# Three-stage kernel: the last expert tile's step takes over the preparation of the dense stage, and four smaller moves

## The chip, the cores and the metric

The kernel runs on one core of one Trainium2 chip, as one program. The metric is the device time of one execution in microseconds (us), and the median of three executions stands for the kernel. TensorE is called PE in the rows, VectorE DVE, ScalarE ACT, GpSimd POOL and SyncE SP. SP only issues transfers. "q" behind an engine's name means its sequencer, the part that reads instructions, tests conditions, loads registers and hands work to the engine.

## The reference

Three layers follow each other. Attention with a window of 16 positions and block summaries gives 1536 tokens of 512 values. A top-1 mixture of 8 experts takes each token through one expert. A dense layer with a squared ReLU ends it.

```python
def reference(**kwargs):
    ...
    attn_out = _attn_ref(**attn_kwargs)          # (2, 8, 768, 64), local window + block maxima and means
    x = attn_out.transpose(0, 2, 1, 3).reshape(B * S, H * D)     # 1536 x 512
    x = _moe_ref(x=x, **moe_kwargs)
    return _moe2_ref(x=x, **moe2_kwargs)

# experts: D 512, F 1024, E 8
logits = x @ w_gate + modality_bias[modality_id]
e_idx = argmax(logits); gate_w = softmax(logits)[e_idx]
out[mask] = gate_w[mask, None] * (relu(x[mask] @ w1[e]) @ w2[e])
# dense: 512 -> 2048 -> 512
h = relu(x @ w_in);  return (h * h) @ w_out
```

## The kernel before

**Stages.** Attention handles the 1536 tokens in 12 blocks of 128 (NB = 12, index i). While it ends, the tokens are routed: each block is scattered to a list of its expert in DRAM (`xs_d`). The expert stage then goes through tiles of 128 tokens, each of one expert; their number n_t is known only at run time (it was 13 in the profiled execution, from 13 times 8 matmuls of one line). The dense stage takes the tokens in 3 groups of 512.

**Precision.** Every fp32 operand is split in two parts, `high` (a copy by ACT) and `low` (the difference, by DVE or POOL), and each product is made of three matmuls. So weights that arrive in `raw` have to be split into `W` before PE can use them. W has two slots. A run is a row of tiles of one expert, and the runs take turns in the slots. The weights come in 8 parts of 512 KB, four of the first layer and four of the second (PARTS = 4). The dense stage's weights go the same way: `w_in` as if it was one more run, and `w_out` into the slot that the last expert leaves, first half (`out_high` and `out_low` of parts 0 to 3) before the dense stage, second half inside it where `swapped` is 0.

**A tile's step** on PE is `layer1(t)`, `x_transpose(t+1)`, `layer2(t-1)`, `h_transpose(t)`. The first three tiles (SPEC = 3) are written out, the others run in a loop of 9 rounds of two steps, each under a test `t < n_t`, on PE, ACT, DVE and SP alike. Rounds past n_t still are gone through, with both tests failing. A last `layer2(n_t - 1)` stands behind the loop. In such a step ACT makes ReLU, `x_high(t+1)`, the high part of h, stores the tile before (`ys_d`), and splits weights where the table says so (`split_next`, which loads a register from `table` and tests it). DVE makes `x_low(t+1)`, `y_copy(t-1)`, `h_low(t)`, and the low parts of weights (`low_next`, which loads and tests likewise).

**Tokens of the dense stage.** Group 0 is read back in four blocks, `z_part[0..3]`, of which the last two lie in `x_in` and are loaded once the last `x_transpose` has run. DVE multiplies each by its gate (`scale_parts`), PE transposes it (`part_transposes`), ACT and DVE split it into `z_hi` and `z_lo`. The first matmuls of the dense stage (`up(0, 0)`) wait for all four `z_lo`. `up(g, f)` is 12 matmuls, followed from f = 2 on by `down(g, f - 2)` of 12; ACT makes `r_sb` from each, DVE `sq`, ACT `s_hi`, DVE `s_lo`, for which `down` waits.

**Order.** Nothing is scheduled by a tool: every engine runs its own instruction list in the order in which it is written, and semaphores join them. Transfers of SP wait in SP's own order.

**The start of the expert stage.** SP loads the first expert's 8 parts of weights from attention's block 9 on. POOL scatters the blocks in five groups (`RGROUPS`); when groups 0 and 1 have landed it reads tiles 0 and 1 from `xs_d` (semaphores `s_x0`), and PE transposes tile 0. `tables()` on DVE makes all per-tile tables and raises `tab`; n_t is read from them. The first matmuls of tile 3 stand behind DVE's `x_low(3)`.

Of the kernel before, what the change touches and what calls it, by code (L numbers as in the profile page):

```python
# [5 lines left out]
F32 = mybir.dt.float32  # L6
# [8 lines left out]
P = 128  # L15
# [36 lines left out]
GT = 4  # L52
# [90 lines left out]
def build(nc, a):  # L143
# [257 lines left out]
    with block:  # L401

        @block.sync
        def _(sp):
# [46 lines left out]
            for i in range(VRING, NB):  # L451
# [35 lines left out]
            with sp.Fori(0, (TILES - SPEC) // 2) as m:  # L487
                for j in range(2):
                    t = m * 2 + (j + SPEC)
                    with sp.If(t < n_t):  # L490
                        moe_step(t, 1 - j)
# [25 lines left out]
        def _(act):  # L517
# [100 lines left out]

            def moe_step(t, s=None, before=None):
# [34 lines left out]
            n_run = n_r(act)  # L654
            with act.Fori(0, (TILES - SPEC) // 2) as m:
                for j in range(2):
                    t = m * 2 + (j + SPEC)
                    with act.If(t < n_t):
                        moe_step(t, j, m + (j + 2))


            swapped = act.snap((n_run + 1) & 1)

            def out_high(part):
                act.activation(Wv(swapped, 0, part * PW, PW), raw[:, part * PW:(part + 1) * PW], ACT.Copy
                               ).then_inc(sem["wo_h"], 1)

            def out_second(parts):
                act.wait_ge(sem["l2"], n_t)
                act.wait_ge(s_wo[1], 16)  # L670
                for part in parts:
                    out_high(part)
# [6 lines left out]
            for j in range(GT):  # L679
                act.wait_ge(sem["zt"], j + 1)  # L680
                act.activation(z_hi[:, :, j * P:(j + 1) * P], part_bank(j)[:, :].rearrange("p (k t) -> p k t", k=KD),
                               ACT.Copy).then_inc(sem["zh"], 1)
            act.wait_ge(sem["l1"], n_t * 2)
            act.wait_ge(s_wo[0], 16)
            for part in range(PARTS):
                out_high(part)
# [183 lines left out]
        def _(dve):  # L870
# [159 lines left out]
            for i in range(NB):  # L1030
# [19 lines left out]
                if i in (5, 6):  # L1050
                    sum_values(1, i - 3)
# [49 lines left out]

            T1 = TILES + 1
# [47 lines left out]
            def moe_step(t, s, lap):  # L1150
                x_low(t + 1)
                if isinstance(t, int) and t == 1:
                    dve.wait_ge(sem["scat_d"], RGROUPS[4][1] * 16)
                dve.wait_ge(s_ys[s], lap * 16 + 16)
                y_copy(t - 1, y_sb[s])
                if isinstance(t, int) and t == 1:
                    rows_of_tiles()
                if not isinstance(t, int):
                    with dve.If(t == last):
                        scale_parts(range(2))  # L1160
                h_low(t)
                if not isinstance(t, int):
# [3 lines left out]
            def scale_parts(js):  # L1166
                dve.wait_ge(sem["sorted"], 16)
                for j in js:
# [41 lines left out]
            dve.tensor_tensor(lsub[:, :, :], logit[:, :, :], wide(lmax[:, :], 2, E), ALU.subtract).then_inc(sem["lsub"], 1)  # L1210
# [17 lines left out]
            with dve.Fori(0, (TILES - SPEC) // 2) as m:  # L1228
                for j in range(2):
                    t = m * 2 + (j + SPEC)  # L1230
                    with dve.If(t < n_t):
                        moe_step(t, j, m + 1)
# [12 lines left out]
            swapped = dve.snap((n_run + 1) & 1)  # L1245

            def out_low(parts):
                for part in parts:
                    dve.wait_ge(sem["wo_h"], part + 1)
                    dve.tensor_tensor(Wv(swapped, 1, part * PW, PW), raw[:, part * PW:(part + 1) * PW],  # L1250
# [398 lines left out]
```

## Time and profile before

| what | us |
| --- | --- |
| median of 3 executions | 542.31 |
| lowest, highest | 540.24, 543.75 |
| the profiled execution, whole | 542.34 |
| its span, first to last instruction | 540.70 |
| PE busy in the span | 512.3 (95%) |
| DVE, ACT, POOL busy | 226.6, 186.5, 87.9 |
| mean granted clock of PE | 0.989 of full speed |

The profiled execution took what the median took, and 1.64 us of it lie outside its span. PE is busy in 95% of the span, but matmuls are pipelined and their ends are modelled, so the share alone doesn't tell how much could be won; the gaps between PE's instructions do.

### The profile page before, as it was taken

The page shows a single profiled execution, that of the slowest core. Times are in us where ns is not written, and L with a number is a line of the kernel's source. Part 1 is how long each engine was busy: PE and PEld are TensorE (multiplying, and loading weights), DVE is VectorE, ACT ScalarE, POOL GpSimd, SP SyncE. Part 2 cuts the span into 40 slices and gives each one's busy share as a digit, 9 for nine tenths or more (in the row PEclk, how much of TensorE's full clock was granted, in tenths as well). Part 3 has the DMA queues.
Part 4 walks back from the last instruction along what each step waited for, and adds up shares of the span by engine and source line. Part 5 has one row for each costly group of instructions (what it writes and reads, how often), then busy time and mean ns, then how long its engine had stood idle before and what let it go on. Part 6 is the DMA issues. An engine that isn't in the chain of part 4 may idle for free.

```text
span 540.7 us, 9465 instructions
## 1 busy us (share of the span) xinstructions
PE 512.3 (95%) x3118; PEld 412.9 (76%) x3119; DVE 226.6 (42%) x439; ACT 186.5 (34%) x353; POOL 87.9 (16%) x111
## 2 busy tenths in 40 slices
PE   8699989979999999997999999999999999999994
PEld 3477778867888888885788888888888888888883
DVE  3686676876312635312862322432332233222231
ACT  0856664315422545421641222332212133122220
POOL 4343335117530040400000000110000020000002
PEclk9989998999999999999999999999999999999998
DMA  8999882229491247531010000120000010000002
GB/s 295 299 269 292 245 287 112 80 52 359 65 334 50 78 178 290 175 133 58 31 68 0 1 1 1 69 86 0 0 0 0 0 58 19 0 0 0 0 0 78
DMA packets 18682, 54.92 MB, mean 102 GB/s; under 512 B 2768, under 2 KB 3040, under 8 KB 17888
## 3 DMA queue, kind: packets, MB, share of 16 engines
q1 hardware_dynamic: 10864, 27.47, 17.0%
q0 software_dynamic: 5200, 23.62, 12.1%
q10 hardware_dynamic: 2592, 3.49, 1.8%
q8 instruction: 15, 0.25, 0.2%
q14 instruction: 11, 0.09, 0.1%
HBM read 42.51 MB, written 12.07 MB: 101 GB/s over the span
## 4 chain that ended last, share of the span: by engine, by line
PE 85%; DVE 5%; issue 3%; DMA 2%; ACT 1%; DVEq 1%; POOL 0%; another core or an unknown queue 0%; POOLq 0%; SPq 0%; ACTq 0%
PE psum L1579 8%; PE psum L1580 8%; PE psum L1578 8%; PE psum L1595 8%; PE psum L1594 8%; PE psum L1596 8%; PE psum L1494 4%; PE psum L1493 4%; PE psum L1495 4%; PE psum L1473 4%; PE psum L1475 4%; PE psum L1474 4%; PE psum L1398 2%; PE psum L1503 2%; PE psum L1313 2%
## 5 line engine op out<-in xcount | busy, mean ns | idle before, releaser
L1268 DVE TENSOR_TENSOR sq<-r_sb 128x512 f32<-128x512 f32 x48 | 33.2, 692 | 137.0 <-ACT r_sb L694 137.0
L694 ACT ACTIVATE r_sb<-psum 128x512 f32<-128x512 f32 x48 | 28.7, 597 | 147.4 <-PE psum L1580 147.4
L1594 PE MATMUL psum<-W,s_hi 128*128 128x512 f32 x192 | 75.8, 395 | 0.0
L1579 PE MATMUL psum<-z_lo,W 128*128 128x512 f32 x192 | 75.8, 395 | 0.0
L1580 PE MATMUL psum<-z_hi,W 128*128 128x512 f32 x192 | 75.8, 395 | 0.0
L1578 PE MATMUL psum<-z_hi,W 128*128 128x512 f32 x192 | 75.7, 394 | 0.0
L1595 PE MATMUL psum<-W,s_hi 128*128 128x512 f32 x192 | 75.6, 394 | 0.0
L1596 PE MATMUL psum<-W,s_lo 128*128 128x512 f32 x192 | 75.3, 392 | 0.0
L860 POOL DMA_INDIRECT out<-o_sb,sorted_m x12 | 11.6, 968 | 297.8 <-ACT o_sb L706 294.8
L1270 DVE TENSOR_TENSOR s_lo<-sq,s_hi 128x512 fp32r<-128x512 f32 x48 | 33.3, 693 | 33.5 <-ACT s_hi L696 33.5
L1473 PE MATMUL psum<-W,x_hi 128*128 (+1 forms) x104 | 42.4, 407 | 1.8 <-issue 1.2
L696 ACT ACTIVATE s_hi<-sq 128x512 fp32r<-128x512 f32 x48 | 30.3, 632 | 38.9 <-DVE sq L1268 38.9
L1578 PEld LDWEIGHTS psum<-z_hi,W 128*128 128x128 f32 x192 | 36.0, 188 | 8.7
L1580 PEld LDWEIGHTS psum<-z_hi,W 128*128 128x128 f32 x192 | 36.0, 187 | 8.7
L1579 PEld LDWEIGHTS psum<-z_lo,W 128*128 128x128 f32 x192 | 36.0, 187 | 8.6
L1594 PEld LDWEIGHTS psum<-W,s_hi 128*128 128x128 f32 x192 | 36.1, 188 | 8.3
L1596 PEld LDWEIGHTS psum<-W,s_lo 128*128 128x128 f32 x192 | 36.1, 188 | 8.2
L1595 PEld LDWEIGHTS psum<-W,s_hi 128*128 128x128 f32 x192 | 36.1, 188 | 8.1
L1493 PE MATMUL psum<-W,h_hi 128*128 (+1 forms) x104 | 41.9, 403 | 0.0
L1475 PE MATMUL psum<-W,x_lo 128*128 (+1 forms) x104 | 41.2, 396 | 0.0
L1474 PE MATMUL psum<-W,x_hi 128*128 (+1 forms) x104 | 41.0, 394 | 0.0
L1494 PE MATMUL psum<-W,h_hi 128*128 (+1 forms) x104 | 40.9, 394 | 0.0
(204 smaller groups left out, 735.5 us busy)
## 6 DMA issues: line engine op xcount, KB each, us to landing
raw<-in_w POOLq DMA_DIRECT2D x4, 2048.0 KB
raw<-in_w_io POOLq DMA_DIRECT2D x4, 2048.0 KB, 8.1
v_in<-in_v SPq DMA_DIRECT2D x12, 390.0 KB, 9.3
raw<-in_w SPq DMA_DIRECT2D x8, 512.0 KB, 8.1
kT<-in_kT SPq DMA_DIRECT2D x8, 400.0 KB, 6.5
q_in<-in_q SPq DMA_DIRECT2D x12, 256.0 KB, 7.9
X<-in_vT SPq DMA_DIRECT2D x2, 1536.0 KB, 13.6
x_in<-xs_d SPq DMA_DIRECT2D x12, 256.0 KB
```

The lines of the kernel that those rows point to most:

```text
L1270: dve.tensor_tensor(s_lo[f % SBUFS][:, :], sq[:, :], s_hi[f % SBUFS][:, :].bitcast(F32), ALU.subtract).then_inc(sem["s_l"], 1)
L1473: pe.matmul(bank[h][:, :], x_hi[:, k, :], wh, start=(k == 0), stop=False)
L1474: pe.matmul(bank[h][:, :], x_hi[:, k, :], wl, start=False, stop=False)
L1475: ins = pe.matmul(bank[h][:, :], x_lo[:, k, :], wh, start=False, stop=(k == KD - 1))
L1493: pe.matmul(bank[4][:, :], h_hi[:, k, :], wh, start=(k == 0), stop=False)
L1494: pe.matmul(bank[4][:, :], h_hi[:, k, :], wl, start=False, stop=False)
L1578: pe.matmul(bank[f % 2][:, :], wh, z_hi[:, k, :], start=(k == 0), stop=False)
L1579: pe.matmul(bank[f % 2][:, :], wh, z_lo[:, k, :], start=False, stop=False)
L1580: ins = pe.matmul(bank[f % 2][:, :], wl, z_hi[:, k, :], start=False, stop=(k == KD - 1))
L1594: pe.matmul(bank[2 + j][:, :], s_hi[f % SBUFS][:, tok], wh, start=(f == 0), stop=False)
L1595: pe.matmul(bank[2 + j][:, :], s_hi[f % SBUFS][:, tok], wl, start=False, stop=False)
L1596: ins = pe.matmul(bank[2 + j][:, :], s_lo[f % SBUFS][:, tok], wh, start=False, stop=(f == KFF - 1))
```

## The change

It has six parts. (1) The last tile's step now holds, under a test `t == last`, what stood behind the loop: on ACT the high parts of group 0's tokens (`parts_high`) and of w_out's first half (`out_first`), on DVE the scaling of all four blocks ahead of `y_copy`, then their low parts, w_out's low parts and the copy of the last y. On PE all 16 transposes of the blocks stand ahead of the last `layer2`, where 8 stood ahead of it and 8 inside. (2) In the loop the second step's test is nested in the first's, so that a round past the end is left after one test. (3) SP issues parts 4 to 7 of the first expert's weights only once tile 1 (`s_x0[1]`) has landed. (4) PE transposes tile 3 inside `layer2(1)`, ahead of its seventh piece of eight, and reads n_t and n_run ahead of its eighth. (5) One reduction of v for the second batch (`sum_values(1, 3)`) moves on DVE from block 6 to block 5. (6) `lsub`, the input of ACT's exponentials of the gates, is computed ahead of the tables.

```diff
@@ SP
-                if i >= NB - RING:
+                if NB - RING <= i < NB - 1:
                     load_weights(e, (i - (NB - RING)) * 2)
-            load_weights(e, 2 * RING)
+            sp.wait_ge(s_x0[1], 16)
+            load_weights(e, PARTS)
+            load_weights(e, PARTS + 2)
@@ ACT
+            def out_first():
+                act.wait_ge(sem["l1"], n_t * 2)
+                act.wait_ge(s_wo[0], 16)
+                out_high(range(PARTS))
...
+            def parts_high():
+                for j in range(GT):
+                    act.wait_ge(sem["zt"], j + 1)
+                    act.activation(z_hi[:, :, j * P:(j + 1) * P], part_bank(j)[:, :].rearrange("p (k t) -> p k t", k=KD),
+                                   ACT.Copy).then_inc(sem["zh"], 1)
...
                 if not isinstance(t, int):
+                    with act.If(t == last):
+                        parts_high()
+                        out_first()
+                if not isinstance(t, int):
                     split_next(t - 1, 1)
                     split_next(t, 0)
...
             with act.Fori(0, (TILES - SPEC) // 2) as m:
-                for j in range(2):
-                    t = m * 2 + (j + SPEC)
-                    with act.If(t < n_t):
-                        moe_step(t, j, m + (j + 2))
+                t = m * 2 + SPEC
+                with act.If(t < n_t):
+                    moe_step(t, 0, m + 2)
+                    with act.If(t + 1 < n_t):
+                        moe_step(t + 1, 1, m + 3)
@@ DVE
-                if i in (5, 6):
-                    sum_values(1, i - 3)
+                if i == 5:
+                    sum_values(1, 2)
+                    sum_values(1, 3)
...
+            dve.tensor_tensor(lsub[:, :, :], logit[:, :, :], wide(lmax[:, :], 2, E), ALU.subtract).then_inc(sem["lsub"], 1)
             T1 = TILES + 1
...
             def moe_step(t, s, lap):
                 x_low(t + 1)
+                if not isinstance(t, int):
+                    with dve.If(t == last):
+                        scale_parts()
...
                 y_copy(t - 1, y_sb[s])
...
+                h_low(t)
                 if not isinstance(t, int):
                     with dve.If(t == last):
-                        scale_parts(range(2))
-                h_low(t)
-                if not isinstance(t, int):
+                        parts_low()
+                        out_low(range(PARTS))
+                        y_copy(last, y_last)
                     low_next(t - 1, range(PARTS, PARTS + 2))
                     low_next(t, range(PARTS))
...
-            scale_parts(range(2, GT))
-            for j in range(GT):
-                dve.wait_ge(sem["zh"], j + 1)
...
-            out_low(range(PARTS))
-            y_copy(last, y_last)
@@ PE
-            x_transpose(3, 1, 1)
-            layer2(1, 0, 1)
+            counts = []
...
+            layer2(1, 0, 1, between=((6, lambda: x_transpose(3, 1, 1)), (KF - 1, load_counts)))
             h_transpose(2)
...
-            part_transposes(range(2))
-            layer2(n_t - 1, swapped, n_run, between=((3, lambda: part_transposes(range(2, GT))),))
+            part_transposes()
+            layer2(n_t - 1, swapped, n_run)
```

On PE, around the second layer of tile 1, before the change. L1430 is a transpose of the tile in `x_in`, L1473 to L1475 are the first layer, L1493 to L1495 the second, L1503 transposes h, and `TENSOR_LOAD` reads a count into a register:

```order
L1475 MATMUL psum<-W,x_lo 128x512
L1430 MATMUL psum<-ident,x_in_155 128x128 [waits s_xs1]
L1430 MATMUL psum<-ident,x_in_155 128x128 x3
L1493 MATMUL psum<-W,h_hi 128x512 [waits s_slbv,s_y,s_hl]
...
L1503 MATMUL psum<-ident,h_sb 128x128 [waits s_relu]
L1503 MATMUL psum<-ident,h_sb 128x128 x3
L343 TENSOR_LOAD table [waits s_tab]
L340 TENSOR_LOAD table
L1527 UNCONDITIONAL_BRANCH
```

The same place with the change (there the transposes of x are L1446, the second layer L1509 to L1511, those of h L1519):

```order
L1491 MATMUL psum<-W,x_lo 128x512
L1509 MATMUL psum<-W,h_hi 128x512 [waits s_slbv,s_y,s_hl]
...
L1446 MATMUL psum<-ident,x_in_155 128x128 [waits s_xs1]
L1446 MATMUL psum<-ident,x_in_155 128x128 x3
L1509 MATMUL psum<-W,h_hi 128x512 [waits s_slbp]
L1510 MATMUL psum<-W,h_hi 128x512
L1511 MATMUL psum<-W,h_lo 128x512
L343 TENSOR_LOAD table [waits s_tab]
L340 TENSOR_LOAD table
L1509 MATMUL psum<-W,h_hi 128x512
```

The wait for tile 3 (`s_xs1`) moved behind 18 matmuls of the second layer, and the two register loads with the wait for `tab` moved ahead of its last three.

On DVE, the second step of a loop round from `x_low` on and what stands behind the loop, before the change (L1174 to L1176 are `low_next`, L1170 the scaling, L1133 a copy of y):

```order
L987 TENSOR_TENSOR x_lo<-psum,x_hi 128x512 [waits s_x_h]
L1133 COPY y_sb_162<-psum 128x512 [waits s_l2,s_ys1]
L1159 COMPARE_AND_BRANCH
L1170 TENSOR_SCALAR z_part_174<-z_part_174,sorted_m 128x512 [waits s_part0,s_sorted]
L982 TENSOR_TENSOR h_lo<-psum,h_hi 128x512 [waits s_hh]
L1174 TENSOR_LOAD table
...
L1228 REGISTER_ALU
L1228 COMPARE_AND_BRANCH
L1170 TENSOR_SCALAR x_in_154<-x_in_154,sorted_m 128x512 [waits s_part2,s_sorted]
L1170 TENSOR_SCALAR x_in_155<-x_in_155,sorted_m 128x512 [waits s_part3]
```

The same step with the change (L1200 is the scaling, L1193 `z_lo`, L1187 w_out's low parts, L1147 a copy of y, L1204 `low_next`, L1258 the loop's end):

```order
L999 TENSOR_TENSOR x_lo<-psum,x_hi 128x512 [waits s_x_h]
L1167 COMPARE_AND_BRANCH
L1200 TENSOR_SCALAR z_part_174<-z_part_174,sorted_m 128x512 [waits s_part0,s_sorted]
L1200 TENSOR_SCALAR x_in_155<-x_in_155,sorted_m 128x512 [waits s_part3]
...
L994 TENSOR_TENSOR h_lo<-psum,h_hi 128x512 [waits s_hh]
L1193 TENSOR_TENSOR z_lo<-psum,z_hi 128x4x128 [waits s_zh] x4
L1187 TENSOR_TENSOR W<-raw,W 128x1024
L1147 COPY y_last<-psum 128x512 [waits s_l2]
L1204 TENSOR_LOAD table
L1258 REGISTER_ALU
```

All that stood behind the loop now stands in the step, ahead of `low_next` and of the rounds past the end, and the wait of the last copy of y for PE's last second layer (`s_l2`) with it.

## Rows read from the trace of the kernel before

**Rows 1.** The page's chain that ended last, by engine.
```profile
PE 85%; DVE 5%; issue 3%; DMA 2%; ACT 1%; DVEq 1%; POOL 0%; another core or an unknown queue 0%; POOLq 0%; SPq 0%; ACTq 0%
```

**Rows 2.** Waits of PE: releaser, us in total, times, longest.
```profile
PE psum L1430 <- DMA x_in<-xs_d: 3.8, 2, 2.3
...
PE psum L1393 <- DVE vsT L900: 1.1, 1, 1.1
```

**Rows 3.** Timeline of DVE at block 5: start, us, work.
```profile
44.22 0.94 DVE L900 TENSOR_REDUCE vsT<-X 128x24 f32<-128x768 f32 x1
```

**Rows 4.** Chain in order of time, between the second scatter and tile 0.
```profile
69.49 6.84 DMA xs_d<-X,dest
...
77.88 2.89 DMA x_in<-xs_d
```

**Rows 5.** SP: last weight loads in the timeline; wait for the last scatters; landing.
```profile
66.98 1.92 SPq L432 DMA_DIRECT2D raw<-in_w  x4
...
SPq L477 <- DMA xs_d<-X,dest: 4.4, 1, 4.4
...
raw<-in_w SPq DMA_DIRECT2D x8, 512.0 KB, 8.1
```

**Rows 6.** Timeline of DVE and ACT in tile 0.
```profile
83.08 0.68 DVE L987 TENSOR_TENSOR x_lo<-psum,x_hi 128x512 fp32r<-128x512 f32 x1
...
92.09 2.00 ACT L560 ACTIVATE W<-raw 128x1024 fp32r<-128x1024 f32 x2
```

**Rows 7.** Windows of 1 us: busy by engine, PE's clock, DMA share, GB/s.
```profile
82.00:83.00 1.00, 1.00 (x23) 0.88 (x19) 1.00 (x2) 1.00 (x2) 0.69 (x1) 0.52 0.00 0
...
84.00:85.00 1.00, 1.00 (x4) 0.81 (x4) 0.97 (x3) 0.00 (x0) 0.69 (x2) 0.50 0.41 160
85.00:86.00 1.00, 1.00 (x5) 0.83 (x4) 0.93 (x1) 0.00 (x0) 0.69 (x2) 0.77 0.42 152
```

**Rows 8.** Timeline of PE and DVE from tile 2's first layer to tile 3's.
```profile
117.66 0.66 PE L1430 MATMUL psum<-ident,x_in 128*128 128x128 f32 x4 [2.33 <-DMA x_in<-xs_d]
118.07 0.48 PE L1493 MATMUL psum<-W,h_hi 128*128 128x512 f32 x1
...
123.67 1.03 PE L1503 MATMUL psum<-ident,h_sb 128*128 128x128 f32 x8
125.89 0.49 PE L1473 MATMUL psum<-W,x_hi 128*128 x1 [1.19 <-issue]
...
123.11 0.69 DVE L987 TENSOR_TENSOR x_lo<-psum,x_hi 128x512 fp32r<-128x512 f32 x1
```

**Rows 9.** Timeline of PE from the last loop step to the dense stage.
```profile
250.94 1.08 PE L1547 MATMUL psum<-ident,z_part 128*128 128x128 f32 x8 [1.41 <-DVE z_part L1170]
...
257.19 1.09 PE L1547 MATMUL psum<-ident,x_in 128*128 128x128 f32 x8 [2.92 <-DVE x_in L1170]
...
261.58 0.39 PE L1578 MATMUL psum<-z_hi,W 128*128 128x512 f32 x1
```

**Rows 10.** The same stretch on ACT, DVE and SP.
```profile
255.99 1.08 ACT L681 ACTIVATE z_hi<-psum 128x512 fp32r<-128x512 f32 x2 [5.77 <-issue]
...
258.86 3.90 ACT L665 ACTIVATE W<-raw 128x1024 f32 x4
...
260.27 4.63 DVE L1250 TENSOR_TENSOR W<-raw,W 128x1024 f32 x4 [0.35 <-ACT W L665]
...
265.43 0.68 DVE L1268 TENSOR_TENSOR sq<-r_sb 128x512 f32<-128x512 f32 x1
266.81 0.69 DVE L1270 TENSOR_TENSOR s_lo<-sq,s_hi 128x512 fp32r<-128x512 f32 x1 [0.70 <-ACT s_hi L696]
...
243.17 0.80 SPq L500 DMA_DIRECT2D x_in<-ys_d  x2
```

**Rows 11.** Chain in order of time: DVE's sequencer in rounds past the end.
```profile
253.40 0.04 DVEq L1228
...
254.41 0.04 DVEq L1228
```

More of the change, by code:

```diff
@@ L654, in _ @@
             n_run = n_r(act)
+            last = act.snap(n_t - 1)
+            swapped = act.snap((n_run + 1) & 1)
             with act.Fori(0, (TILES - SPEC) // 2) as m:
-                for j in range(2):
-                    t = m * 2 + (j + SPEC)
-                    with act.If(t < n_t):
-                        moe_step(t, j, m + (j + 2))
[L662 to L672, printed above, removed]
+                t = m * 2 + SPEC
+                with act.If(t < n_t):
+                    moe_step(t, 0, m + 2)
+                    with act.If(t + 1 < n_t):
+                        moe_step(t + 1, 1, m + 3)
             def z_high(g):
@@ L1228, in _ @@
             with dve.Fori(0, (TILES - SPEC) // 2) as m:
[L1229 to L1232, printed above, removed]
+                t = m * 2 + SPEC
+                with dve.If(t < n_t):
+                    moe_step(t, 0, m + 1)
+                    with dve.If(t + 1 < n_t):
+                        moe_step(t + 1, 1, m + 1)
             def scale(g):
@@ L1243, in z_low @@
                                       ).then_inc(sem["zl"], 1)
[L1245 to L1250, printed above, removed]
-                                      Wv(swapped, 0, part * PW, PW).bitcast(F32), ALU.subtract).then_inc(sem["wo_v"], 1)
-            scale_parts(range(2, GT))
-            for j in range(GT):
-                dve.wait_ge(sem["zh"], j + 1)
-                dve.tensor_tensor(z_lo[:, :, j * P:(j + 1) * P], part_bank(j)[:, :].rearrange("p (k t) -> p k t", k=KD),
-                                  z_hi[:, :, j * P:(j + 1) * P].bitcast(F32), ALU.subtract).then_inc(sem["zl"], 1)
-            out_low(range(PARTS))
-            y_copy(last, y_last)
             with dve.If(swapped == 1):
@@ L1509, in weights_of, with moe_step @@
                 return pe.snap(both & 1), pe.snap(both >> 1)
+            def moe_step(t, s, lapx):
+                last = []
+                layer1(t, *weights_of(t), between=((KD // 2, lambda: last.extend(weights_of(t - 1))),))
+                x_transpose(t + 1, s, lapx)
+                layer2(t - 1, *last)
+                h_transpose(t)
             layer1(0, 0, 1, between=((1, tail_a), (2, tail_b), (3, tail_c), (KD, tail_d)))
@@ L1540, in _, with part_transposes @@
             first_half = pe.snap(swapped * (2 * PARTS) + AHEAD)
-            def part_transposes(js):
-                for j in js:
+            def part_transposes():
+                for j in range(GT):
                     pe.wait_ge(sem["scale"], j + 1)
```

57 lines of the change are left out of this document (34 added, 23 removed).

## The prediction

> **What bounds the kernel now.** I read the chain first: PE is 85% of it, DVE 5%, bare issue 3%, transfers 2% [rows 1]. So the time is PE's work, which the change leaves as it is, plus the gaps between pieces of it. Next come PE's waits: 3.8 us for tiles from DRAM in two waits, the longest 2.3, and 1.1 us for a reduction of v [rows 2]. The timeline adds 1.19 us of bare issue ahead of tile 3 [rows 8] and two gaps of 1.41 and 2.92 us at the loop's end [rows 9]. In between, the steps of the loop stand without gaps. Last come the windows: PE ran at 0.52 and 0.50 of its clock around 82 to 85 us and at 0.77 in the next, busy all the time [rows 7]. So all there is to win lies in four places, some 10 us of gaps and 1.7 us of clock; I go through them in order of time.
>
> **Part 5, the reduction of v.** PE waits 1.1 us for the fourth sum [rows 2]; one such reduction takes 0.94 us on DVE [rows 3]. It is now done a block earlier, at the cost of as much there. Nothing in the rows says that PE waits for DVE in that block; if all of it lay open, the gain would be nothing. Bounds: 0 to 1.1. I take 0.9, because PE's wait list has no entry of DVE's maxima, for which the moved work would make room. From here to the scatters everything follows in the chain, so the 0.9 is carried on.
>
> **Part 3, weights later.** SP issues parts 4 to 7 (2 MB) from 66.98 to 68.90, and each part takes 8.1 us to land [rows 5]. The scatter of 69.49 therefore shares the transfer engines with all of them and takes 6.84 us; the read of tile 0 follows at 77.88 and takes 2.89 [rows 4]. The scatter that landed with the weights gone shows what is left of it: SP waited 4.4 us for the last ones [rows 5]. So tile 0 lands up to 6.84 - 4.4 = 2.4 us earlier. PE is there 3.8 - 2.33 = 1.5 us before it [rows 2, 8], so of the 2.4 only 1.5 can be used. I take 1.4, bounds 0.5 (part of parts 0 to 3 still in flight) and 1.5.
>
> With the gap, the slow clock may go. At 0.52, 0.50, 0.50 (the window between reads like its neighbours) and 0.77 of the clock the four microseconds from 82 lost 0.48 + 0.50 + 0.50 + 0.23 = 1.7 us against a full clock [rows 7]. The granted clock is at the lower of its two levels, 1.2 GHz, and fell just behind the wait for tile 0. Part of this can't be won, since PE then stands before DVE's first `x_low`, of 83.08 [rows 6]; I take 1.2, bounds 0 and 1.7.
>
> The Trainium skill says, in "TensorE: Matmul & The Clock Gate", section "Part 4: PE-mode transpose", that transposes don't count as a busy PE for the clock. The stretch ahead of 82 us is full of transposes, so by that rule the clock falls with or without the gap; that is the first rival below.
>
> The price of part 3: the parts now land some 8 us behind tile 1. POOL reads tile 1 right behind tile 0, which then lands at 78 to 79. SP then needs 1.9 us for four issues, and at 8.1 us each they land by 84 to 89 [rows 4, 5]. The part that is needed soonest with work behind it is the sixth: ACT splits parts 5 and 6 from 92.09 on, and tile 0's ReLU stands behind them [rows 6]. With everything up to 3.5 us earlier that is 88.6. It is close, and I cost it at nothing; bounds 0 and 2.
>
> **Parts 4 and 6, tile 3.** Tile 2's first layer ends at 117.66 - 2.33 = 115.3. Then PE waits for tile 3. With the change 18 of the second layer's 24 matmuls come first. 24 take 123.67 - 118.07 = 5.60 us [rows 8], or 0.233 each, so 18 take 4.2: PE is at 119.5, behind the landing of 117.66. Four transposes (0.41), six matmuls (1.4) and eight transposes (0.9) follow: 122.2. The two register loads hide behind the matmuls ahead of them; they were most of the 1.19 us of issue. What is late next is DVE: `x_low(3)` runs from 123.11 to 123.80 at the end of the tables [rows 8], and `lsub` moves within DVE's list, so its sum is the same. Tile 3's first matmul goes from 125.89 to 123.9: 2.0 us. Bounds: 1.0 (if the loads show after all), and 3.5 (both gaps in full, if `x_low(3)` came earlier too, for which I see no reason). ACT no longer waits for `lsub`, which keeps its ReLU of tile 2 ahead of the new, earlier transposes of h; without it the 2.0 would be lost.
>
> **Parts 1 and 2, the loop's end.** 13 tiles use 5 of 9 rounds, so 4 rounds are run through empty, at 254.41 - 253.40 = 1.01 us each [rows 11], on every engine. A round has three jumps, and now two: I take 0.67 for it, 1.3 us less in all (bounds 0.5 and 2.0). PE ends the step at 250.94 - 1.41 = 249.5 and starts on the blocks at 250.94 [rows 9]; with 1.3 less it starts at about 249.6. 8 transposes take 1.0 us, 16 take 2.0: 251.6. The last second layer takes 5.60: 257.2. ACT no longer runs the empty rounds ahead of `z_hi` (it stood at 255.99 after 5.77 us of issue [rows 10]); four of them at 0.54 end at 253.3 and the last `z_lo` at about 254, well before. So the dense stage starts at 257.2, not 261.58 [rows 9]: 4.4 us.
>
> The price is on DVE. ACT's four high parts take 3.90, so from 253.3 to 257.2; DVE's four low parts take 4.63 from the first of them on [rows 10], so to about 259.3. Then `y_copy(last)`, two register loads (0.7 each, if three of them and a loop's start cost PE the 1.19 of issue and some hidden time [rows 8]), and four rounds of 0.67: DVE is free for the first `sq` at about 263.5. In the rows `s_lo` is ready 266.81 + 0.69 - 265.43 = 2.07 us behind the start of `sq` [rows 10], so at 265.6. The first `down` follows 36 matmuls of 0.233 behind the start, at 265.6. That is even; before, 261.58 + 8.4 against 267.5, it had 2.5 us to spare. I take 0.4 us off: 4.0, bounds 2.5 and 4.6. Scaling all four blocks ahead of `y_copy` costs nothing: the last two are issued from 243.17 to 243.97 [rows 10], and DVE has until the second layer in that step ends, some 248.5 (249.5 less the 1.03 of the transposes of h).
>
> **Sum.** 0.9 + 1.4 + 1.2 + 2.0 + 4.0 = 9.5 us. 542.34 - 9.5 = 532.8, and since the profiled execution took the median of the runs (542.31), that is the forecast for the median too. The bounds add up to gains of 4.0 - 2 for late weights, and 12.4 at most, so 540 and 530.
>
> **Rivals.**
> The clock falls anyway. For it: the clock is low while PE is fully busy, and the stretch before is transposes and narrow matmuls; against it: it fell right behind a gap. It gives 1.2 us back: 534.0.
> DVE becomes the bound at the dense stage's start. For it: it has no slack in my sum, and a round may still cost 1.01 us (4 times 0.34 more, on PE too). The first `down` then waits 1.4 + 1 us more: 535.2.
> The late weights hold ACT. For it: four parts and four scatters of the same time share the engines. Against: most of the list above has slack. ACT then keeps tile 0's ReLU for 2 us, and the gain at the start and of the clock is largely lost: 537.
> Slower than before: the test around a longer body makes a jump, in each of the 10 loop steps, that reaches beyond what the sequencer holds, and PE stands in every step. In the rows a round that jumps takes 1.01 us; steps with work show no gap. If each of the 10 steps stood for 1.5 us, that is +15: 547.8. It decides from 1 us a step. Against it: PE's own list is no longer than before. The Trainium skill, "Runtime: NRT & Kernel Launch", section "Instruction fetch mechanics", says that a taken branch outside the fetched pages waits for a transfer; no row here shows that on PE.
> The change doesn't do what it says: if the last tile stood first in its round, `last` would still be found, so I see only the case that gaps reopen elsewhere: 541.
>
> **How the numbers follow.** Forecast 0.45, clock 0.23, DVE 0.14, late weights 0.12, slower 0.03, nothing 0.03. A measurement of this kernel tells about 1%, 5.4 us, from no change. The first three cases and half of the fourth lie below 536.9: 0.85 faster with some left for errors common to all; same 0.12; slower 0.03. For the range, 529.8 takes in the upper bounds, and 537.8 the late weights.
>
> **What the changed profile would show.** PE's transpose of tile 0 with no wait, or one under 0.3 us, and a granted clock of 1.00 around 80 to 85. No wait ahead of the transposes of tile 3, and its first matmul right behind an `x_low`. From the last h transposes to the first matmul of the dense stage 7.7 us in place of 12.0, with 16 transposes in a row. A short PE wait for DVE's `s_lo` ahead of the first `down`, or none. The forecast is wrong if ACT's split of parts 5 and 6 waits for a transfer, if PE's steps are longer than the 12.5 us that 48 matmuls and 12 transposes make, or if DVE's first `sq` comes later than 7 us behind the start of the dense stage.

## The result

The changed kernel takes 533.6 us in the median of 4 executions (532.38 to 535.28), against 542.47 us for the kernel before in the same comparison: a ratio of 0.983, 95% interval 0.980 to 0.986, or 8.9 us. Run again later, beside 23 executions of the kernel before, it gave 0.986 (0.980 to 0.991), 8.3 us. The forecast was 532.8, with a range of 529.8 to 537.8. The profiled execution took 533.67 us, 532.0 of it its span, and the rows below are from it.

The chain's shares by engine, from the page:

```profile
PE 89%; DVE 5%; issue 1%; DMA 1%; ACT 1%; POOL 1%; DVEq 0%; ACTq 0%; POOLq 0%
```

PE had 85% of it before, and issue 3% [rows 1]. Next PE's waits, where those of [rows 2] stood:

```profile
PE psum L1320 <- ACT prob L540: 3.9, 3, 2.0
PE psum L1489 <- DVE x_lo L999: 1.7, 2, 1.1
PE psum L1519 <- ACT h_sb L649: 1.7, 1, 1.7
...
PE psum L1446 <- DMA x_in<-xs_d: 0.3, 1, 0.3
```

The waits for tiles fell from 3.8 to 0.3 us, the one for the fourth sum of v is gone, and the one for ACT's `h_sb` grew: before it was 0.5. The start shows where it comes from. First the timeline of SP, PE and ACT, then one line of the chain, then windows of 1 us (columns as in [rows 7]):

```profile
77.89 1.92 SPq L432 DMA_DIRECT2D raw<-in_w  x4
...
76.57 0.63 PE L1446 MATMUL psum<-ident,x_in 128*128 128x128 f32 x4 [0.32 <-DMA x_in<-xs_d]
...
90.86 1.09 PE L1519 MATMUL psum<-ident,h_sb 128*128 128x128 f32 x8 [1.71 <-ACT h_sb L649]
...
90.12 1.09 ACT L649 ACTIVATE h_sb<-psum 128x512 f32<-128x512 f32 x2 [1.13 <-DMA xs_d<-X,dest]
```

```profile
82.72 7.38 DMA xs_d<-X,dest
```

```profile
82.00:83.00 1.00, 1.00 (x5) 0.81 (x5) 0.83 (x6) 0.98 (x2) 0.69 (x2) 1.00 0.90 277
...
85.00:86.00 1.00, 1.00 (x19) 0.93 (x17) 0.00 (x0) 0.00 (x0) 0.00 (x0) 1.00 1.05 416
...
92.00:93.00 1.00, 1.00 (x24) 0.98 (x22) 0.75 (x4) 1.00 (x3) 0.00 (x0) 0.50 0.00 0
93.00:94.00 1.00, 1.00 (x4) 0.73 (x3) 0.86 (x7) 0.62 (x1) 0.43 (x1) 0.50 0.00 0
94.00:95.00 1.00, 1.00 (x4) 0.81 (x3) 1.00 (x1) 0.00 (x0) 0.69 (x2) 0.50 0.00 0
```

Tile 0 is there almost at once, and the clock stays at its upper level (2.4 GHz) where it was at 0.50 to 0.77 before [rows 7]. But the late weights now share the engines (DMA share 0.90 and 1.05) with the scatter of 82.72. That scatter takes 7.38 us, ACT's ReLU of tile 0 waits for it, PE waits 1.71 us for ACT, and the clock falls to its lower level (1.2 GHz) just behind that wait. So in this execution the jam of [rows 4] and [rows 5] was moved, not removed.

Tile 3, PE's timeline (before: [rows 8]):

```profile
118.38 0.50 PE L1509 MATMUL psum<-W,h_hi 128*128 128x512 f32 x1 [0.41 <-issue]
119.18 1.04 PE L1519 MATMUL psum<-ident,h_sb 128*128 128x128 f32 x8
121.36 0.49 PE L1489 MATMUL psum<-W,x_hi 128*128 x1 [1.13 <-DVE x_lo L999]
```

The loop's end on PE, ACT and DVE (before: [rows 9, 10]):

```profile
243.97 1.03 PE L1519 MATMUL psum<-ident,h_sb 128*128 128x128 f32 x8
244.96 1.08 PE L1570 MATMUL psum<-ident,z_part 128*128 128x128 f32 x8
245.88 1.04 PE L1570 MATMUL psum<-ident,x_in 128*128 128x128 f32 x8
...
252.59 0.39 PE L1601 MATMUL psum<-z_hi,W 128*128 128x512 f32 x1
...
246.36 2.07 ACT L640 ACTIVATE z_hi<-psum 128x512 fp32r<-128x512 f32 x4 [0.66 <-PE psum L1570]
248.28 3.92 ACT L624 ACTIVATE W<-raw 128x1024 f32 x4
...
254.25 0.69 DVE L1147 COPY y_last<-psum 128x512 f32<-128x512 f32 x1
258.79 0.69 DVE L1284 TENSOR_TENSOR sq<-r_sb 128x512 f32<-128x512 f32 x1 [3.85 <-issue]
260.18 0.69 DVE L1286 TENSOR_TENSOR s_lo<-sq,s_hi 128x512 fp32r<-128x512 f32 x1 [0.70 <-ACT s_hi L708]
```

All 16 transposes stand in a row without a gap, and the dense stage starts 8.62 us behind the last transposes of h, in place of 13.08. DVE's rounds past the end (3.85 us of issue) are now what its first `sq` waits for. `s_lo` is ready at 260.87, and the first `down` is at 261.22, where 36 matmuls alone would have put it at 261.0.

### The profile page after: what moved, and what is told of

Read it like the earlier page. It is cut to its first block, busy times and chain, and to the rows that moved or that the text cites. A ratio compares the mean times of both kernels' runs of the same rounds, so it can differ in the third digit from the quotient of the medians.

```text
span 532.0 us, 9413 instructions
## 1 busy us (share of the span) xinstructions
PE 511.1 (96%) x3118; PEld 412.3 (78%) x3119; DVE 226.1 (42%) x439; ACT 186.5 (35%) x353; POOL 87.5 (16%) x111
## 4 chain that ended last, share of the span: by engine, by line
PE 89%; DVE 5%; issue 1%; DMA 1%; ACT 1%; POOL 1%; DVEq 0%; ACTq 0%; POOLq 0%
PE psum L1603 8%; PE psum L1602 8%; PE psum L1601 8%; PE psum L1617 8%; PE psum L1618 8%; PE psum L1619 8%; PE psum L1509 4%; PE psum L1510 4%; PE psum L1511 4%; PE psum L1489 4%; PE psum L1491 4%; PE psum L1490 4%; PE psum L1329 2%; PE psum L1354 2%; PE psum L1414 2%; PE psum L1519 2%
## 5 line engine op out<-in xcount | busy, mean ns | idle before, releaser
L1509 PE MATMUL psum<-W,h_hi 128*128 (+1 forms) x104 | 42.0, 404 | 0.5 <-issue 0.4
```

What stands on the lines that cost most here:

```text
L1509: pe.matmul(bank[4][:, :], h_hi[:, k, :], wh, start=(k == 0), stop=False)
```

## The experiments

Whole times of kernels that differ by 1 to 2 us overlap, since executions of one kernel spread over 3 to 8 us. So each profile is cut into stretches at PE's checkpoints. A is the start of tile 2's first layer. B is from there to tile 3's first layer, C from there to the last transposes of h, D from there to the dense stage. The last column is the part of A behind M, the start of PE's last mask matmuls (`cb`, 128x480), which belong to attention's block 11. The kernel before issues the weights that part 3 moves at 66.98 us [rows 5], about when PE is at M, so part 5 acts ahead of M and part 3 behind it.

| kernel | A | B | C | D | A from M |
| --- | --- | --- | --- | --- | --- |
| before | 109.56 | 16.33 | 122.61 | 13.08 | 41.39 |
| before, again | 109.56 | 16.75 | 123.21 | 14.68 | 41.26 |
| before + part 3 | 107.36 | 16.64 | 122.61 | 14.68 | 41.39 |
| before + part 6 | 113.42 | 15.32 | 124.15 | 13.08 | 43.56 |
| after | 106.92 | 14.44 | 122.61 | 8.62 | 41.45 |
| after, again | 109.04 | 14.43 | 122.63 | 8.60 | 39.23 |
| without part 3 | 110.22 | 14.43 | 122.61 | 8.70 | 44.47 |
| parts 6, 7 late only | 107.16 | 14.46 | 122.64 | 8.65 | 42.91 |
| without part 5 | 108.74 | 14.44 | 122.61 | 8.62 | 40.59 |
| without part 1 | 107.20 | 14.44 | 125.45 | 11.91 | 40.58 |
| without part 2 | 112.19 | 14.42 | 125.30 | 9.79 | 40.38 |
| without part 4 | 108.95 | 15.20 | 124.56 | 8.74 | 39.09 |
| without part 6 | 106.61 | 14.79 | 125.14 | 8.74 | 39.35 |
| `x_low(3)` early | 107.71 | 13.23 | 123.25 | 8.74 | 40.39 |

B and D repeat within 0.15 us where neither the clock nor the code of the stretch differs. A doesn't, and C has a disturbance of up to 2.8 us; both are told in the last section. One disturbance of A matters for what follows. Around 60 us ACT stops with no releaser in the trace, in both profiles of the kernel before but not in the first of after (first ACT before, then PE at M before and after):

```profile
60.21 0.60 ACT L556 ACTIVATE xT<-psum 128x512 f32<-128x512 f32 x1 [2.95 <-remote]
...
68.17 0.56 PE L1304 MATMUL psum<-cb 128*128 128x480 bf16 x2
...
65.47 0.56 PE L1320 MATMUL psum<-cb 128*128 128x480 bf16 x2
```

The stop is in nine of the fourteen profiles. PE's step from one block to the next around it takes 6.9 us with the stop. Without the stop it takes 5.1 us in kernels without part 5, and 5.7 in kernels with it. The first four experiments ran together (before: 542.72 us, 17 executions), the next four too (544.98, 22), and the last four (544.66, 23). Ratios, not times, compare across these.

**Part 3 undone.** Weights 4 to 7 are issued in block 11 again.

```diff
-                if NB - RING <= i < NB - 1:
+                if i >= NB - RING:
                     load_weights(e, (i - (NB - RING)) * 2)
-            sp.wait_ge(s_x0[1], 16)
-            load_weights(e, PARTS)
-            load_weights(e, PARTS + 2)
+            load_weights(e, 2 * RING)
```

> The changed kernel with part 3 undone: the first expert's parts 4 to 7 are issued early again. Theory A (part 3 only moves the contention): in the changed kernel it won about 1.1 us at the wait for tile 0 and 1.2 us of clock, and lost 1.7 us at tile 0's ReLU, which waited for a scatter that took 7.38 us beside the weights, and 1.2 us of clock behind that wait. So without it the time is that of the changed kernel within 0.6 us, 533.0 to 534.2; the wait for tile 0 is back to 1.2 to 1.5 us with a low clock behind it, and the wait ahead of the first transposes of h is 0.5 us. Theory B (my prediction's sum: part 3 is worth 2.6 us): 536.2.

Measured: 536.3 us, ratio 0.989 (0.984 to 0.993). PE is earlier than before at tile 0's place, so a landing at the same time makes a longer wait, and the clock falls during it (timeline, then windows of 2 us):

```profile
80.97 1.09 PE L1444 MATMUL psum<-ident,x_in 128*128 128x128 f32 x4 [4.43 <-DMA x_in<-xs_d]
```

```profile
80.00:82.00 2.00, 1.03 (x6) 0.73 (x6) 0.00 (x0) 0.00 (x0) 1.82 (x2) 0.50 0.23 92
82.00:84.00 2.00, 2.00 (x34) 1.88 (x34) 0.69 (x1) 1.55 (x2) 1.39 (x3) 0.50 0.39 152
84.00:86.00 2.00, 2.00 (x8) 1.82 (x9) 1.89 (x4) 0.00 (x0) 1.57 (x2) 0.61 0.63 242
```

Behind M this profile takes 44.47 us, against 41.45 and 39.23 in the two profiles of after, so part 3 is worth 3 us or more there: theory B. By the whole times it is 1.5 to 2.9 us (0.989 against 0.986 and 0.983), with intervals that overlap. Without it A is even 0.7 us later than in the kernel before, although part 5 is in.

**Part 3 alone**, on the kernel before, the same edit the other way round.

```diff
-                if i >= NB - RING:
+                if NB - RING <= i < NB - 1:
                     load_weights(e, (i - (NB - RING)) * 2)
-            load_weights(e, 2 * RING)
+            sp.wait_ge(s_x0[1], 16)
+            load_weights(e, PARTS)
+            load_weights(e, PARTS + 2)
```

> The kernel before with part 3 alone. Theory A: 542.5 within 0.8 us, since what it wins at tile 0 it loses at tile 0's ReLU; the profile shows both. Theory B: 539.9. A third reading, that the missing 1.9 us stop of DVE and ACT near 58 us in the changed kernel comes from part 3's lighter transfer load, would show here as no stop near 58 us and a time 1.2 us lower than either.

Measured: 542.4 us, ratio 1.001 (0.998 to 1.003): nothing, as theory A has it. PE's two waits in this profile, for tile 0 and for the ReLU of tile 0 (1.43 and 0.46 us in `before`):

```profile
77.90 1.09 PE L1432 MATMUL psum<-ident,x_in 128*128 128x128 f32 x4 [1.13 <-DMA x_in<-xs_d]
...
92.53 1.06 PE L1505 MATMUL psum<-ident,h_sb 128*128 128x128 f32 x8 [1.45 <-ACT h_sb L627]
```

A is 2.2 us earlier than before, but all of that stands ahead of M (65.97 against 68.17), where part 3 can't act: 1.8 us are the stop around 60 us, which this profile lacks, and 0.4 stand there by 45 us. From M on both take 41.39 us. PE wins 0.30 us at the one wait and loses 0.99 at the other, and the clock is at 0.50 for as long (3.4 us, here from 78 to 81). The third reading in the expectation, that part 3 takes the stop away, fails: the kernel without part 3 lacks the stop too.

The clock also falls at 115 to 119 and 255 to 259 us, behind the waits for tile 3 and for `x_in` at the loop's end, as in the second profile of the kernel before and not in the first. That isn't what hides a gain either. As an estimate from each execution's span and mean granted clock, the lower clock took 9.2 us of this kernel in the median and 9.5 of the kernel before beside it. Why part 3 wins nothing alone and 3 us in company stays open. The rows show only that PE comes to tile 0 at 79.5 us in `before` and at 76.5 in the kernel without part 3, and that its transpose starts at 80.9 in both.

**Half of it**: only parts 6 and 7 wait for tile 1.

```diff
-                if NB - RING <= i < NB - 1:
+                if i >= NB - RING:
                     load_weights(e, (i - (NB - RING)) * 2)
             sp.wait_ge(s_x0[1], 16)
-            load_weights(e, PARTS)
-            load_weights(e, PARTS + 2)
+            load_weights(e, 2 * RING)
```

> The changed kernel with only parts 6 and 7 issued late (1 MB instead of 2). Theory A: both scatters see half the contention; tile 0 lands some 1 us later than in the changed kernel (a wait of 0.3 to 1.3 us), the ReLU's wait shrinks from 1.1 us to nothing, and if one of the two low-clock stretches goes too, 532.0 to 533.0. If both stay, 533.5. Theory B: halfway between 536.2 and 533.6, 534.9.

Measured: 535.21 us, ratio 0.987 (0.983 to 0.992). PE waits 2.19 us for tile 0 and the clock is low from 76.5 to 83.3 us, but ACT's ReLU of tile 0 no longer waits for a scatter. A is 0.24 behind the full change. Behind M it takes 42.91 us, halfway between 44.47 and 41.45, as theory B has it, but one profile each can't tell the two halves apart.

**Part 5 undone**: `sum_values(1, 3)` is back in block 6.

```diff
-                if i == 5:
-                    sum_values(1, 2)
-                    sum_values(1, 3)
+                if i in (5, 6):
+                    sum_values(1, i - 3)
```

> The changed kernel with part 5 undone: the fourth sum of v is made in block 6 again. Prediction's term: 0.9 us, so 534.5. The traces of before and after differ by 1.24 us more than at the start across PE's wait for that sum: 534.8. Rival: the whole 2.7 us that PE is earlier at block 9 belongs to it, because the stop of DVE and ACT near 58 us comes back with it: 536.3. If the time doesn't move, other slack downstream took the gain.

Measured: 535.82 us, ratio 0.987 (0.983 to 0.992). PE's wait of 1.07 us for `vsT` is back. A is 1.8 us behind the full change and 0.3 ahead of its repetition, which the clock and the stop decide. The step of PE in which the sum stands tells more: 6.72 us, against 5.47 with part 5. Two steps on, part 5 gives 0.57 of that back (5.68 in place of 5.11), but only where the stop around 60 us is absent. So this part is worth 0.7 us without the stop and 1.2 with it.

**Part 1 undone**: the preparation stands behind the loop again; the tests stay nested.

```diff
-                    with act.If(t == last):
-                        parts_high()
-                        out_first()
...
+            parts_high()
+            out_first()
...
-            part_transposes()
-            layer2(n_t - 1, swapped, n_run)
+            part_transposes(range(2))
+            layer2(n_t - 1, swapped, n_run, between=((3, lambda: part_transposes(range(2, GT))),))
```

> The kernel after with part 1 undone: the high and low parts of the dense stage's tokens and of w_out's first half stand behind the loop again, on PE 8 transposes ahead of the last second layer and 8 inside it; the nested tests (part 2) stay. Theory A (the jump of the empty rounds is what stood in the way, and both parts share the gain): DVE and ACT come out of the loop some 1.3 us earlier than before, but still run four empty rounds (4 x 0.7 us) with the preparation behind them, so PE waits some 1 us ahead of the second half of the transposes, and the dense stage starts 257.5 - 255.5 us in: 536.5 (535.5 to 537.5). Theory B (nesting alone is worth nothing, all of the loop's end is part 1): 538.0, the whole 4.2 to 4.5 us back. Rival C (nesting alone does it): 534.5 or less.

Measured: 538.89 us, ratio 0.987 (0.981 to 0.992). PE still waits 1.79 us for the second half of the blocks, and ACT's sequencer walks through the empty rounds ahead of `z_hi` (4.82 us of issue, 5.77 before). D is 11.91: theory A, with a smaller share for the nesting.

**Part 2 undone**: the two tests side by side again on all four engines.

```diff
-                t = m * 2 + SPEC
-                with dve.If(t < n_t):
-                    moe_step(t, 0, m + 1)
-                    with dve.If(t + 1 < n_t):
-                        moe_step(t + 1, 1, m + 1)
+                for j in range(2):
+                    t = m * 2 + (j + SPEC)
+                    with dve.If(t < n_t):
+                        moe_step(t, j, m + 1)
```

> The kernel after with part 2 undone: the two tests of a round stand side by side again on SP, ACT, DVE and PE, so that a round past the end runs through both. Theory A: a round costs PE and DVE about 0.3 us more, 4 rounds 1.3 us. PE has a gap of about 1.4 us behind the last step's h transposes where the kernel after has about 1.0 or less, and DVE reaches its first squaring of the dense stage 1.3 us later, so the first down waits about that: 534.5 to 535.2. Rival B: PE's empty rounds are passed while it still works off queued matmuls, and DVE's first squaring has slack: 533.6, within 0.4.

Measured: 538.92 us, ratio 0.991 (0.987 to 0.994), the largest loss of the four together. PE's waits from 250 to 275 us, and DVE's first `sq`:

```profile
PE psum L1566 <- issue: 1.4, 1, 1.4
PE psum L1613 <- DVE s_lo L1283: 1.2, 1, 1.2
```

```profile
269.03 0.69 DVE L1281 TENSOR_TENSOR sq<-r_sb 128x512 f32<-128x512 f32 x1 [5.36 <-issue]
```

DVE's issue is 5.36 us in place of 3.85, 0.38 for each of 4 rounds. From the last transposes of h to the first `down` it is 19.55 us, 17.25 with part 2. Against the kernel before (21.47) part 2 alone gives 1.16, seen in the kernel without part 1 (20.31), and part 1 alone 1.92. Both give 4.22. The last 1.1 us are there only with both: with the empty rounds behind the preparation, what is left of them decides when DVE reaches `sq`.

**Part 4 undone**: tile 3 is transposed ahead of `layer2(1)`, and the counts are read behind the transposes of h.

```diff
-            layer2(1, 0, 1, between=((6, lambda: x_transpose(3, 1, 1)), (KF - 1, load_counts)))
+            x_transpose(3, 1, 1)
+            layer2(1, 0, 1)
             h_transpose(2)
+            load_counts()
```

> The kernel after with part 4 undone: tile 3 is transposed ahead of layer2(1), and n_t and n_run are read behind the transposes of h. Theory A (the sizes of the prediction's term): PE waits 2 to 3 us for tile 3's load, then 1.2 us of bare issue ahead of tile 3's first layer, whose first matmul comes at 123.2 in place of 121.4: 535.5 (534.9 to 536.2). Theory B (lsub alone made the change there, as ACT is no longer held): under 534.2. Rival C: the gap lowers the clock as it did around tile 0, and the gain is larger than its gaps: over 536.5, with a granted clock of 0.5 to 0.7 behind the wait.

Measured: 537.57 us, ratio 0.986 (0.982 to 0.989). PE waits 2.38 us for the tile as before, but the 1.19 us of issue do not come back, and B is only 0.76 longer: less than the 1.8 of theory A. No fall of the clock stands behind this wait, so rival C isn't seen here. Its first layer follows the transposes at once:

```profile
117.11 0.66 PE L1446 MATMUL psum<-ident,x_in 128*128 128x128 f32 x4 [2.38 <-DMA x_in<-xs_d]
...
123.11 1.03 PE L1519 MATMUL psum<-ident,h_sb 128*128 128x128 f32 x8
124.15 0.49 PE L1489 MATMUL psum<-W,x_hi 128*128 x1
```

**Part 6 undone**: `lsub` is back behind the tables and DVE's register loads.

```diff
-            dve.tensor_tensor(lsub[:, :, :], logit[:, :, :], wide(lmax[:, :], 2, E), ALU.subtract).then_inc(sem["lsub"], 1)
             T1 = TILES + 1
...
             swapped = dve.snap((n_run + 1) & 1)
+            dve.tensor_tensor(lsub[:, :, :], logit[:, :, :], wide(lmax[:, :], 2, E), ALU.subtract).then_inc(sem["lsub"], 1)
```

> The kernel after with part 6 undone: lsub stands behind the tables and the register loads of DVE again, so ACT's exponentials of the gates start at about 118 in place of 112.5 us, and with them its ReLU of tile 2 and the high part of tile 3. Theory A: PE's transposes of h of tile 2, at 119.5 in the kernel after, wait for that ReLU for 1 to 2 us, or DVE's low part of tile 3 comes later by as much: 534.9 (534.2 to 536.0), with a wait for ACT's h_sb or x_hi in PE's list. Rival B: ACT's list has slack there and PE waits for nothing: 533.6, within 0.4.

Measured: 536.84 us, ratio 0.984 (0.980 to 0.989). ACT's ReLU of tile 2 ends at 119.62, PE waits 0.18 us for it, and B is 0.35 longer. Theory A's wait is there at about a quarter of its price (0.35 of 1.3 us).

**Part 6 alone**, on the kernel before.

```diff
+            dve.tensor_tensor(lsub[:, :, :], logit[:, :, :], wide(lmax[:, :], 2, E), ALU.subtract).then_inc(sem["lsub"], 1)
             T1 = TILES + 1
...
-            dve.tensor_tensor(lsub[:, :, :], logit[:, :, :], wide(lmax[:, :], 2, E), ALU.subtract).then_inc(sem["lsub"], 1)
```

> The kernel before with part 6 alone: lsub ahead of the tables. Theory A (the bare issue of 1.19 us ahead of tile 3's first layer was there because PE's sequencer stood at the transposes of h until ACT, held by lsub, had made its ReLU at 122.6, and only then read its two registers): ACT's ReLU of tile 2 comes at about 115, the issue is gone, and tile 3's first matmul stands 15.2 us behind tile 2's in place of 16.3: 541.3 (540.7 to 541.9). Rival B (the register loads cost their 1.2 us wherever they stand behind the transposes): 542.4, the issue unchanged.

Measured: 544.13 us, ratio 0.999 (0.996 to 1.002): too small for the whole time. In the profile theory A holds: B is 15.32, and the 1.19 us of issue are gone. In the kernel before PE's sequencer stood at the transposes of h until the ReLU of 122.6 and only then read its registers; the loads cost nothing once nothing holds it.

**Both kernels again**, unchanged.

> The kernel after, unchanged, once more. Four profiled executions of its neighbours show ACT and DVE standing for some 7 us around 132 to 138 us with no releaser in the trace, at a price of about 2.5 us, and the profile of the kernel after doesn't. Theory A (it belongs to the execution, not to the edit): the times of this kernel spread over 532 to 538 too, its median is 1.5 to 2.5 us above 533.6, and its profile may show the same stop. Theory B (it belongs to the edits): 533.6, within 0.7, with no stop.

> The kernel before, unchanged, once more, for a second profile. Theory A: the stop of ACT and DVE that its first profile shows around 58 to 60 us comes and goes between executions, and another may stand around 132; every other number (wait for tile 0 2 to 2.9, tile 3 2.3, issue 1.2, loop's end 13.1 us from the last transposes of h to the dense stage) stays within 0.3. Theory B: the same trace as the first within 0.3 us throughout.

Measured: 536.37 us for after (532.74 to 539.03), ratio 0.986; 544.78 for before, ratio 1.002 (0.998 to 1.005). The median of after is 2.8 us above the first one, but the kernel before beside it rose by 2.2, so this says little. Its profile has no stop around 132 us, and has the one around 60 us that the first lacks, so that one belongs to the execution, as theory A says of such stops. For before theory A holds, with the clock's falls on top of what it said: its "within 0.3" did not hold at the loop's end (14.68 against 13.08).

**An edit of my own**: in the kernel after DVE makes `x_low(3)` right behind its register loads.

```diff
             swapped = dve.snap((n_run + 1) & 1)
+            x_low(3)
```

> The kernel after with one edit of its own: DVE makes x_low of tile 3 right behind its register loads, at 118.4, and not behind the ten small operations on positions and gates, at 120.2. Theory A (DVE's list is what bounds tile 3's first layer in the kernel after, with a wait of 1.13 us for x_lo): the wait goes and the first matmul follows the transposes of h, 13.3 us behind tile 2's in place of 14.4: 532.5 (531.9 to 533.2). Rival B (ACT's high part of h of tile 2 or the split of the next weights is then late, or the small operations hold POOL's stores): the 1.1 us come back as a wait further on, 533.6.

Measured: 535.74 us, ratio 0.985 (0.981 to 0.990), and 0.6 us under the kernel after beside it, which is within the spread. B is 13.23, as theory A has it, but C and D give back 0.64 and 0.14 of the 1.2: ACT's split of the next weights waits for its transfer in both kernels, `x_low(4)` stands behind that split on DVE, and PE now stands for 0.37 us ahead of tile 4's first layer. The trace calls that issue; `x_low(4)` ended 0.46 us ahead of the matmul, about as `x_low(3)` does where PE waits for it (0.50), so it is the likely cause. Some 0.4 us remain, which these runs can't confirm.

## Why the prediction was right, and where not

**Loop's end, 4.4 less 0.4: measured 4.46, and 4.22 at the first `down`.** The steps on PE and ACT came as worked out: 16 transposes in a row, no gap, ACT early, the scaling of all blocks hidden, and DVE's `sq` just late enough to cost 0.24. DVE's own sum has a slip: 259.3 with 0.69 for `y_copy`, 1.4 for the loads and 2.7 for the rounds is 264.1, not 263.5. The `sq` came 6.20 us behind the dense stage's start, where 263.5 means 6.3, because the work ahead of it ended 0.4 us sooner and the loads and rounds took 3.85 in place of 4.1. That it fitted so well is partly luck. The round's price was right too: 0.34 a round was taken, 0.38 measured. The rival that DVE becomes the bound was true as a mechanism, at 0.24 in place of 2.4 us.

**Tile 3, 2.0: measured 1.89 [rows 8], and what is late next is DVE, as said.** Two reasons given for it were wrong. The register loads were not "most of the 1.19 us of issue": that gap came from `lsub`, which held ACT and so PE's sequencer. And "without it the 2.0 would be lost" fell too, since without part 6 B loses only 0.35. Parts 4 and 6 overlap: DVE's list ends about where each gap did, so either part alone wins 1.0 to 1.5 of the 1.9.

**Start, 0.9 + 1.4 + 1.2 = 3.5: measured 2.64 between the first two profiles, 0.52 between the second two.** M divides it. In the first pair after is 2.70 us ahead at M (65.47 against 68.17). Of that 1.25 is part 5, for which 0.9 was taken, 0.25 was there before, and 1.2 is the stop that `before` has and `after` hasn't. That last piece is chance, and it stood in for the two terms of part 3: behind M the pair takes 41.39 and 41.45 us, so 1.4 + 1.2 came to nothing. In the second pair both have the stop, after is 1.51 us late at M, having lost 3.4 us of clock at 61 to 68 us, and wins 2.03 behind it (41.26 against 39.23), with no wait for tile 0 and no fall. One reading under the term of 1.4 was weak: the 4.4 us taken for a scatter free of the weights are a wait of SP [rows 5], not a scatter's duration.

What failed in the first pair is the price of part 3, "it is close, and I cost it at nothing". The late weights did hold ACT, though not at parts 5 and 6 but through the scatter of 82.72 that ACT's ReLU waits for. PE's new wait of 1.71 us and the clock's fall (1.5 us in the three windows from 92 to 95 us) gave back what part 3 had won. Of the nine profiles with all four parts late this happens in two, `after` and part 3 alone, the two with the earliest M (65.47 and 65.97). In the other seven PE waits 0.45 to 0.47 us for that ReLU, as it did before, and the clock stays at 1.00 from 70 to 110 us. So the rival "late weights hold ACT" was true in some executions, within its bound of 2, together with the forecast.

**The clock** was taken from one profile, at one place. It stayed at 1.00 from 76 to 88 us in the profile of after, in a stretch that holds transposes and narrow matmuls, and fell behind a wait again. So the first rival, that the clock falls there with or without the gap, did not come true. The Trainium skill, "TensorE: Matmul & The Clock Gate", section "Part 4: PE-mode transpose", says that transposes don't count as a busy PE. The stretch up to 79.5 us, transposes and narrow matmuls alone, shows no fall; since the two kinds are mixed in it, no run here tests that rule by itself.

**The sum.** 2.64 + 1.89 + 4.22 = 8.75, and the spans differ by 8.7, for a forecast of 9.5. The loop's end and tile 3 give 6.1 of it for the reasons given. The start is near its term partly by luck, as told above. In the second pair 0.52 + 2.32 + 0.58 + 5.84 = 9.26, and the spans differ by 9.2: less at the start, and more where the gaps of the kernel before cost clock. That cost the sum left out. It is 1.6 us at the loop's end in two of four profiles of kernels that have that gap in full, and none in the ten of kernels that lack it or have it shortened. Over the executions of the last comparison the estimate of what the lower clock took is 8.7 us before and 7.0 after, in the median, so some 1.7 of the 8.3 us are clock.

## What to carry to other kernels

Price a gap with the clock's fall that may follow it, and look at more than one profile before you say that a gap costs none. Ahead of crediting a part with an earlier checkpoint, put a checkpoint where the part can't have acted yet: here that showed 2.2 us of apparent gain to be no gain, but for the most part a stop that one execution had and the other hadn't. When a bare issue stands behind a wait, ask first what held the sequencer at the instruction ahead: here one small operation of DVE, moved, took away what looked like the price of two register loads. A transfer moved out of the way of one reader lands in the way of the next, so list who waits on every transfer of the new time.

## What the runs showed of the hardware

**The clock falls in different places of the same kernel.** Between 40 us and PE's last matmul, the granted clock fell to 0.50 at 82 to 85 us in one profile of before, and in the other at 81 to 84, 118 to 122 and 258 to 262. In after it was 92 to 95 in one and 61 to 68 in the other (3.4 us of loss). Each of these falls but that of the second profile of after begins within 1.2 us of the end of a PE wait of over 1.3 us; that one follows a few short gaps of 0.25 to 0.44 us. In the kernel without part 3 the fall begins some 2.2 us before its wait of 4.43 us is over. The same waits without a fall are in the profiles too (tile 3's wait of 2.33 in the first of before). Two windows of the second profile of before, with the clock near its lower level:

```profile
118.00:120.00 2.00, 2.00 (x9) 1.67 (x8) 1.18 (x8) 0.00 (x0) 0.80 (x1) 0.63 0.00 0
...
260.00:262.00 2.00, 2.00 (x6) 1.52 (x6) 1.26 (x3) 2.00 (x3) 0.00 (x0) 0.53 0.00 0
```

**ACT and DVE stop together, and the trace names no cause.** In the profile of the kernel without part 6 both wait 7 us and go on within 0.01 us of each other, though PE had ended the transposes that ACT needs at 134.1. PE has work until 140 us and then loses about 2.5 us. ACT's and DVE's timeline, then windows of 2 us:

```profile
138.24 1.09 ACT L653 ACTIVATE h_hi<-psum 128x512 fp32r<-128x512 f32 x2 [7.67 <-remote]
...
138.25 0.69 DVE L1146 COPY y_sb<-psum 128x512 f32<-128x512 f32 x1 [6.71 <-remote]
```

```profile
130.00:132.00 2.00, 2.00 (x10) 1.63 (x10) 1.54 (x2) 0.57 (x2) 1.60 (x2) 1.00 1.00 300
132.00:134.00 2.00, 2.00 (x15) 1.75 (x14) 0.00 (x0) 0.00 (x0) 1.49 (x2) 1.00 1.13 62
134.00:136.00 2.00, 2.00 (x11) 1.62 (x10) 0.00 (x0) 0.00 (x0) 1.39 (x3) 1.00 0.29 39
```

The DMA engines count as full at 132 to 134 us while they move 62 GB/s. The stop is in the first pass through the second half of the loop's body in six of fourteen profiles (C is 0.6 to 2.8 us longer there). A like stop of about 3 us on ACT, at 56 to 64 us, is in nine of the fourteen, both of before among them. It is in the second profile of after and not in the first, with the same code, so it isn't made by an edit. The four profiles of the first comparison all lack it and the eight of the later two all have it. The three comparisons ran on different chips, so it may belong to the chip as well as to the execution. The Trainium skill, "Runtime: NRT & Kernel Launch", section "Instruction fetch mechanics", says that the sequencer fetches its instructions by DMA and that a taken branch can wait for that. A fetch held up by full engines would fit both places. No run here tests it, and the instruction packets that the trace shows don't stand at the end of either stop. Near 60 us they stand in the profiles without the stop too (57 to 58 us in the first of after), so the cause stays open.
